# Attention's first step: the order of the first loads, and the bank of unit 0's second group

## What is computed

```
scale = 1 / sqrt(sqrt(D))                     # D = 64, 4 batches x 8 heads, 576 rows, 128 features
phi(x):  h = x @ omega.T - sum(x * x) / 2     # per row
         h = h - max(h)                       # over the 128 features
         return exp(h) / sqrt(128)
q_p, k_p = phi(q * scale), phi(k * scale)
kv  = k_p.T @ v;   z = sum of k_p over rows
out = (q_p @ kv) / (q_p @ z + 1e-6)
x = dense(out):  h = x @ w_in;  (h * sigmoid(1.702 h)) @ w_out
y = experts(x):  the expert with the largest logit, relu, times its gate
```

## Time and profile before

| | |
|---|---|
| median of three runs | 773.05 us (772.09 to 773.67) |
| the profiled execution: its own time | 775.4 us |
| its span, first to last instruction | 773.5 us |
| TensorE matmuls busy | 758.0 us, 98% |
| VectorE, ScalarE, GpSimd busy | 345.8, 315.1, 344.4 us |
| mean granted TensorE clock | 0.997 |

### The profile page before, as it was taken

How to read it: one execution, slowest core, us unless ns; L and a number is a source line. 1 busy time by engine, 2 the same in 40 slices (tenths; PEclk the granted TensorE clock), 3 DMA queues, 4 the chain that set the end, 5 groups by cost and what they waited for, 6 DMA issues and landing times.

```text
span 773.5 us, 15064 instructions
## 1 busy us (share of the span) xinstructions
PE 758.0 (98%) x5332; PEld 677.3 (88%) x5333; DVE 345.8 (45%) x890; ACT 315.1 (41%) x688; POOL 344.4 (45%) x280
## 2 busy tenths in 40 slices
PE   8989999999999999999999999999999999999996
PEld 7978888888888888888888888998999999999996
DVE  6878888211124344234334346783962332332231
ACT  4878888433243223322243223445324325325220
POOL 6788893244212222222232222258727627528421
PEclk9999999999999999999999999999999999999998
DMA  8878882011041000200020000450172613421111
GB/s 333 290 258 283 278 279 88 28 41 42 1 179 40 1 1 0 108 0 0 0 81 29 1 1 0 141 217 29 32 259 92 209 52 123 164 61 31 31 61 33
DMA packets 26169, 75.30 MB, mean 97 GB/s; under 512 B 3200, under 2 KB 4096, under 8 KB 26000
## 3 DMA queue, kind: packets, MB, share of 16 engines
q1 hardware_dynamic: 22432, 64.13, 23.6%
q0 software_dynamic: 3264, 10.03, 4.3%
q10 hardware_dynamic: 432, 0.59, 0.2%
HBM read 61.11 MB, written 13.63 MB: 97 GB/s over the span
## 4 chain that ended last, share of the span: by engine, by line
PE 86%; DVE 5%; issue 3%; DMA 2%; ACT 2%; POOL 1%; SPq 0%; POOLq 0%; DVEq 0%; ACTq 0%
PE pj L772 26%; PE nm L984 14%; PE pj L1438 8%; PE nm L1482 6%; PE kv L984 6%; PE tr L984 6%; PE kv L1482 6%; PE nm L1438 5%; PE pj L269 2%; PE nm L347 2%; PE kv L285 1%; PE pj L1495 1%; DVE pj L537 1%; DMA ve<-in_v_z 1%; PE tr L1434 1%
## 5 line engine op out<-in xcount | busy, mean ns | idle before, releaser
L957 POOL TENSOR_TENSOR gl<-sg,gh 128x512 fp32r<-128x512 f32 (+1 forms) x80 | 94.7, 1184 | 286.8 <-ACT gh L794 286.8
L788 DVE TENSOR_TENSOR sg<-pj,sg 128x512 f32<-128x512 f32 (+1 forms) x80 | 50.9, 637 | 211.5 <-ACT sg L781 211.4
L781 ACT ACTIVATE sg<-pj 128x512 f32<-128x512 f32 (+1 forms) x80 | 44.2, 553 | 140.4 <-PE pj L772 140.2
L772 PE MATMUL pj<-xh,win_h 128*128 128x512 f32 x256 | 100.0, 391 | 0.0
L772 PE MATMUL pj<-xh,win_l 128*128 128x512 f32 x256 | 99.6, 389 | 0.0
L772 PE MATMUL pj<-xl,win_h 128*128 128x512 f32 x256 | 99.6, 389 | 0.0
L794 ACT ACTIVATE gh<-sg 128x512 fp32r<-128x512 f32 (+1 forms) x80 | 47.2, 590 | 100.1 <-PE tr L984 61.1
L1438 PE MATMUL pj<-xTh,W 128*128 128x288 f32 x320 | 71.3, 300 | 0.2 <-DVE xTl L1711 0.2
L918 DVE SCALAR_TENSOR_TENSOR raw<-pj,xT 128x512 f32<-128x512 f32 x96 | 62.5, 689 | 19.7 <-ACT pj L859 13.2
L1242 POOL TENSOR_TENSOR W<-wraw,W 128x1024 fp32r<-128x1024 f32 x28 | 66.3, 2397 | 8.2 <-ACT W L1238 8.2
L772 PEld LDWEIGHTS pj<-xl,win_h 128*128 128x128 f32 x256 | 48.1, 188 | 9.9
(11 more groups left out here) (302 smaller groups left out, 1789.1 us busy)
## 6 DMA issues: line engine op xcount, KB each, us to landing
wraw<-in_moe_w SPq DMA_DIRECT2D x7, 2048.0 KB, 10.4
ve<-in_v_z SPq DMA_DIRECT2D x16, 585.0 KB, 4.7
qk<-in_qk_n SPq DMA_DIRECT2D x15, 576.0 KB, 6.0
qkT<-in_qk_t SPq DMA_DIRECT2D x15, 576.0 KB, 6.8
y_rows<-ys SPq DMA_DIRECT2D x18, 256.0 KB, 2.3
stage<-in_moe_w_in SPq DMA_DIRECT2D x8, 512.0 KB, 6.6
y_early<-ys SPq DMA_DIRECT2D x16, 256.0 KB, 2.9
stage<-in_moe_w_out SPq DMA_DIRECT2D x4, 512.0 KB, 5.9
```

Of the source, the lines that this page charges most:

```text
L772: mm = eng.matmul(ph[f % 3][:, 0:tiles_of(n) * P], w[f // F1A][:, c, f % F1A, :], x[:, c, :], start=(c == 0 and w is win_h and x is bh), s ...
L781: eng.activation(sg[f % 2][:, at], ph[f % 3][:, at], ACT.Sigmoid, scale=1.702).then_inc(a_sg, 1)
L788: eng.tensor_tensor(sg[f % 2][:, at], ph[f % 3][:, at], sg[f % 2][:, at], ALU.mult).then_inc(v_g, 1)
L957: eng.tensor_tensor(gl[f % 3][:, at], sg[f % 2][:, at], gh[f % 3][:, at].bitcast(F32), ALU.subtract).then_inc(g_gl, 1)
```

## The change

The loads get another order. Behind the three thirds of unit 0's `qkT` come unit 0's values, then the first third of unit 1's `qkT` with a semaphore of its own (`ld_t1g0`), then unit 1's `qk`, the other two thirds of its `qkT`, and unit 1's values. Unit 0's second group is projected into `nms` and its third into `pj[0]`, which its first group had; the third therefore waits for the first group's subtraction and exponents. Unit 1's first group goes to `pj[1]`, which no group of unit 0 uses any more, and waits for its own load alone; its second group waits for the rest of `qkT`. The four idle matmuls behind unit 0's third group go, and three stand behind its first and three behind its second.

```diff
--- before.py
+++ after.py
@@ -114,6 +114,7 @@
     ld_w = [sem(f"ld_w{a}") for a in range(2)]
     ld_om = sem("ld_om")
     ld_0, ld_1 = ([sem(f"ld_{b}{g}") for g in range(PG)] for b in range(2))
+    ld_t1 = sem("ld_t1g0")
     g_id = sem("g_id")
     v_om = sem("v_om")
     t_qf = sem("t_qf")
@@ -143,7 +144,10 @@
     def pair_of(i, a, g):
 
 
-        return nms if isinstance(i, int) and i == 0 and g == PG - 1 else pj[(a + g) % 2]
+
+        if isinstance(i, int) and i == 0:
+            return (pj[0], nms, pj[0])[g]
+        return pj[(a + g) % 2]
 
     def sync(eng):
         def load(i, n, a, chunk):
@@ -155,26 +159,31 @@
                 eng.wait_ge(g_sq, 4 * (i - 3) + 1 if isinstance(i, int) else 4 * i - 11)
             eng.dma_start(qk[a][:, :, :].rearrange("p j d -> p (j d)"),
                           qk_n[bass.ds(i, 1), :, :].rearrange("i p r -> (i p) r")).then_inc(ld_qk[a], 16)
+            if isinstance(i, int) and i == 1:
+                n = GT * P
+                eng.dma_start(qkT[1][:, GT:T2, :].rearrange("p t c -> p (t c)"), qk_t[1, :, n:PG * n])\
+                   .then_inc(ld_t[1], 16)
+                return
 
             need(eng, p_pj, PG * (i - 1))
             eng.dma_start(qkT[a][:, :, :].rearrange("p t c -> p (t c)"),
                           qk_t[bass.ds(i, 1), :, :].rearrange("i p r -> (i p) r")).then_inc(ld_t[a], 16)
             if chunk is not None:
                 weights(i - 2, a, chunk)
-            if not (isinstance(i, int) and i == 1):
-                values(i, a)
+            values(i, a)
 
         def values(i, a):
             need(eng, p_kv, i - 1)
             eng.dma_start(ve[a][:, :, :].rearrange("p j c -> p (j c)"),
                           v_z[bass.ds(i, 1), :, :].rearrange("i p r -> (i p) r")).then_inc(ld_v[a], 16)
 
-        def first(g):
+        def first(i, g, done):
+
 
 
             n = GT * P
-            eng.dma_start(qkT[0][:, GT * g:GT * g + GT, :].rearrange("p t c -> p (t c)"),
-                          qk_t[0, :, g * n:(g + 1) * n]).then_inc(ld_0[g], 16)
+            eng.dma_start(qkT[i][:, GT * g:GT * g + GT, :].rearrange("p t c -> p (t c)"),
+                          qk_t[i, :, g * n:(g + 1) * n]).then_inc(done, 16)
 
         def weights(c, a, chunk):
 
@@ -188,10 +197,11 @@
 
         eng.dma_start(om_r[:, :], om_2).then_inc(ld_om, 16)
         for g in range(PG):
-            first(g)
+            first(0, g, ld_0[g])
+        values(0, 0)
+        first(1, 0, ld_t1)
         load(1, 0, 1, None)
-        for i in (0, 1):
-            values(i, i)
+        values(1, 1)
         for i in (2, 3):
             load(i, 1, i - 2, "in")
         for lo, hi, chunk in ((2, NWIN, "in"), (NWIN, NWIN + NWO, "out"), (NWIN + NWO, UNITS - 2, None)):
@@ -257,10 +267,15 @@
 
             if isinstance(i, int) and i == 0:
                 eng.wait_ge(ld_0[g], 16)
+            elif isinstance(i, int) and i == 1:
+                if g == 0:
+                    eng.wait_ge(ld_t1, 16)
+                if g == 1:
+                    eng.wait_ge(ld_t[1], 16)
             elif g == 0:
                 need(eng, ld_t[a], 16 * (n + a))
 
-            if not (isinstance(i, int) and i == 0):
+            if not (isinstance(i, int) and (PG * i + g < 2 or PG * i + g == PG)):
                 need(eng, v_sb, PG * i + g - 1)
                 need(eng, a_exb, PG * i + g - 1)
             pair = pair_of(i, a, g)
@@ -358,9 +373,10 @@
         idle(7)
         eng.wait_ge(v_om, 1)
         project(0, 0, 0, 0)
+        idle(3)
         project(0, 0, 0, 1)
+        idle(3)
         project(0, 0, 0, 2)
-        idle(4)
 
         def step(i, n, a, last):
             x = (i + 1, n + a, 1 - a)
```

## The result

The changed kernel takes 776.31 us (median of 12 runs, 774.62 to 777.76) against 773.59 for the kernel before (12 runs): ratio 1.0037, 95% interval 1.0028 to 1.0046. It is slower by 2.7 us, where 2.0 was forecast. Measured a second time it was slower by 3.3 us (1.0040, 1.0026 to 1.0054).

A forecast was written before the change was run, and what follows sets the result against it. TensorE, busy 98%, bounds the kernel, so early losses move the end; unit 1's `qk`, 1.97 us later, delays its third group. Other costs nothing: 773.05 + 1.97 = 775.0 us, range 772.7 to 776.9.

The forecast's parts named there:

- The place and the mechanism: Unit 1's first step: `qk` queued behind 777 KB more, so squares, `norms` and TensorE's third group start 1.97 us later.
- The hand-over: From unit 1 on, VectorE, ScalarE and TensorE pass the 1.97 us lateness on group by group, without slack.
- The size of the queue's delay: SyncE's queue: unit 1's `qk` lands 1.97 us later, 11.64 instead of 9.67; bounds 1.48 and 2.27.
- Rival D: TensorE's clock falls in the new gap before unit 1's third group, costing 1.7 us more: 776.7 us; chance 0.12.
- the forecast's case: Whole kernel: the 1.97 us shift comes through whole, 775.0 us, own range 774.5 to 775.4; chance 0.55.
- The gap: TensorE before unit 1's third group: done near 14.9 us, then idle until 18.54, 3.6 us.
- The Trainium skill's rule: TensorE in the new gap: an idle array falls to half clock, giving 776.7 us if 3.6 us idle is enough.
- The give-back (B): Units 5 and 6: waits there return the shift in part or whole, 773.9 us, at most 772.8; chance 0.25.
- The reserve of 2.19 us: VectorE's two waits for squares after unit 5's slow `qk` load, 0.92 and 1.27 us, which might absorb lateness.
- The signs named for B and D: Wrong if VectorE's waits at units 5 and 6 fall below 0.92 and 1.27 us, or 1.65 us groups follow 18.5.
- The costs set at nothing: Units 0 and 1: fillers and bank, up to 0.8 us, and unit 1's first group, covered by the wait for `norms`.
- Two bounds: Whole kernel: upper ends 775.4 us for the shift coming through whole and 776.9 with the clock's fall added.

The follow-up runs named there:

- order_only: The change's new order of loads alone, with banks, waits and fillers of the kernel before: 775.59 us, ratio 1.0041 to the kernel before.
- banks_only: The change's banks, waits and fillers alone, with unit 1's `qk` and `qkT` again ahead of unit 0's values: 773.30 us, 1.0005 to the kernel before.
- rows_first: The whole change, but unit 1's `qk` ahead of unit 0's values in the queue: 773.15 us, ratio 1.0006 to the kernel before.
- before_again: The kernel before, unchanged, measured once more for a second profile: 773.25 us, ratio 1.0001.
- change_again: The changed kernel once more, beside its version with fillers on the same chip: 776.37 us, ratio 1.0040 to the kernel before.
- filled twin: The whole change plus ten idle matmuls in TensorE's gap before unit 1's third group: 775.04 us (1.0025 to the kernel before), again 775.28 (1.0023).
- gap_filled_again: Second measurement of the change plus ten idle matmuls in TensorE's gap: 775.28 us, ratio 1.0023 to the kernel before.

## Why the prediction was right

**The place and the mechanism** were right: `qk` behind 777 KB in a queue that answers in order, the squares from there, VectorE's wait, the idle TensorE, and nothing left of the sums' 1.1 us. order_only and banks_only show it by halves, and rows_first, which differs from the change in the place of `qk` alone, is back at the time of before. The hand-over was as tight as forecast, 6.46 us from `norms` to `norms` whatever the lateness.

**The size of the queue's delay** (1.97 us) was right within the spread of the executions, and the runs tell no more than that it is 1.5 to 2.0. The two pairs of profiles, before with after and before_again with change_again, differ by 1.45 and 1.51. With `qk` in its old place seven profiles of five kernels have it landing at 9.67 (before), 9.41 (before_again), 8.72, 9.12, 8.61, 8.17 and 9.47, in the mean 9.0; behind one load of values five have 11.12 (after), 10.92, 11.16, 10.82 and 11.22, in the mean 11.05. That is 2.0 us, the forecast's term; but by the kernel before alone (9.54) it is 1.5, the forecast's lower bound. In the time, the late rows alone are the filled twin's 1.7 and 2.2 us.

**Rival D** had 0.12 and should have had more. It came as a part of the forecast's case and not in its place: 1.1 us of the median (change against filled twin, 776.37 against 775.28), 2.2 us by the two executions with a mean clock of 0.991 against the five with 0.996 or more. That the ten between them had a shorter fall at the same place fits their times, but the mean clock doesn't tell where it was low, and none of the ten has a profile; that stays open.

Nor is a low mean clock found only with the late `qk`. Of 90 executions of the kernel before with a known clock none is below 0.995, but of the eleven of banks_only and the eleven of rows_first two each are at 0.993 or 0.994, and took 774.9 to 775.2 us. Both kernels have TensorE idle for 1.5 to 1.6 us before the sums or the group ahead of them; in their profiles the clock stayed high there, and where it was low in the others is not known.

D's price of 1.7 us came from a low stretch of 3.4 us; the measured one lasted 6.7 and cost 2.5. The 3.4 was a misreading: in the earlier trace rows the low rate began with the first filler and not with the gap before 7.14 (seven fillers in 3.36 us, 0.48 each, where the ten of gap_filled_again take 0.24 each), so it had lasted over 8 us. The gap was forecast at 3.6 us and was 2.5, since TensorE ended its transposes at 15.5 and not 14.9, and `qk` landed 0.5 us before its time. D's term accounts for 2.7 and 3.3 us where 2.0 was forecast: the forecast of the median had the first part of the loss right and left the second to a rival.

**The Trainium skill's rule** (TensorE: Matmul & The Clock Gate, section Part 1) that an idle array falls back to half its clock is borne out by two profiles, after 2.48 and 4.14 us idle, and not by two others, after 2.58 (change_again) and 2.16 (order_only). By it alone the end would have been D's 776.7; it was 776.3.

**The give-back (B)** was read from a stall that the kernel does not have. The reserve of 2.19 us was one execution's, as before_again shows; the median had none of it to give. Its chance of 0.25 was too high, and the 2.35 us by which that execution lay above the median should have been the warning. The signs named for B and D as ones of a wrong forecast, no waits at units 5 and 6 and groups of 1.65 us behind the gap, both showed in the profile after; only the second meant what it was said to mean.

**The costs set at nothing** (fillers, bank, unit 1's first group) were nothing that can be measured: banks_only is at 1.0005 (0.9996 to 1.0014). The second group started at 7.75, 0.6 us later than before, within the 0.8 allowed; the sooner groups hid behind `norms`.

**Two bounds** are not what their terms add up to: 773.05 + 2.27 is 775.3 (775.4 stands there), and with 1.7 more 777.0 (776.9). Nothing hangs on them.

## What to carry to other kernels

Where loads share one queue that answers in order, to bring one forward is to put another back by its bytes over the rate; look which of the two has the longer work behind it before its first use (here 5 us of squares against none). An idle stretch that a late load opens on TensorE can cost twice, once as itself and once as a low clock behind it; fillers that nobody reads separate the two. And where the one profiled execution lies above the median by more than the effect in question, take a second profile before reading a reserve out of its waits.

## What was not expected of the hardware

The clock's fall did not follow the length of the gap alone: idle for 2.48 us it fell, idle for 2.58 us in another execution of the same kernel it did not. Once low it stayed so, in both profiles that show it, through a stretch of 6.7 us of nearly steady work. And the same load at the same place of the queue landed between 8.2 and 9.7 us in seven executions of five kernels, a spread of more than half the effect under study.
